# Attention tables on two engines, w loaded into its table, and SyncE waiting for the last scatters

## The reference

```python
for t in range(S):
    cur = np.einsum('bhd,bhe->bhde', u[None] * kt, vt)
    y[:, :, t] = np.einsum('bhd,bhde->bhe', rt, state + cur)
    state = w[None, :, :, None] * state + np.einsum('bhd,bhe->bhde', kt, vt)
...
skip_score = x @ w_skip; do_compute = skip_score > 0
e_idx = np.argmax(logits, axis=1); gate_w = probs[..., e_idx]
y = gate_w[:, None] * (np.maximum(x[rows of e] @ w1[e], 0) @ w2[e])
```

## Time and profile before

| | us |
|---|---|
| median of 3 runs | 607.92 |
| lowest and highest | 605.97, 608.97 |
| the profiled execution | 608.97 |
| its span, first to last instruction | 607.3 |
| TensorE busy | 559.0 (92%) |
| VectorE busy | 384.1 (63%) |
| GpSimd busy | 251.0 (41%) |
| ScalarE busy | 236.0 (39%) |
| mean granted clock of TensorE | 0.961 of full |

### The profile page before, as it was taken

The page is one execution under the profiler, slowest core; times in us unless marked ns, Lnnn a source line. Parts: engine busy times, 40 slices in busy tenths (PEclk is TensorE's granted clock), DMA queues, the critical chain, the costliest instruction groups (busy, mean ns, idle before and its releaser), DMA issues. The chain is left out here.

```text
span 607.3 us, 15679 instructions
## 1 busy us (share of the span) xinstructions
PE 559.0 (92%) x5618; PEld 532.4 (88%) x5619; DVE 384.1 (63%) x762; ACT 236.0 (39%) x567; POOL 251.0 (41%) x346
## 2 busy tenths in 40 slices
PE   3999999989799999999949779999999999999993
PEld 3899889968799999999938669999999999999992
DVE  5898888958777777777714745564647463737330
ACT  0233333324166565556605014362526351516220
POOL 5777778721443334443330033141524332324231
PEclk9899999987799999999979798999999999999997
DMA  9698899766377567666459111545264434111100
GB/s 141 105 188 159 160 167 166 144 248 209 123 248 229 164 219 242 216 190 189 123 147 361 35 50 47 200 137 192 71 223 159 149 138 148 48 40 44 39 15 25
DMA packets 114123, 89.54 MB, mean 147 GB/s; under 512 B 80672, under 2 KB 104931, under 8 KB 114080
## 3 DMA queue, kind: packets, MB, share of 16 engines
q1 hardware_dynamic: 106304, 74.16, 43.6%
q0 software_dynamic: 7776, 14.82, 8.8%
HBM read 80.44 MB, written 13.27 MB: 154 GB/s over the span
## 5 line engine op out<-in xcount | busy, mean ns | idle before, releaser
L814 DVE TENSOR_TENSOR w_lo<-w_raw,w_hi 128x384 fp32r<-128x384 f32 (+1 forms) x224 | 130.3, 608 | 6.2 <-ACT w_hi L809 2.4
L1079 PE MATMUL e_ps_h<-e_x_hi,w_hi 128*128 128x256 f32 (+2 forms) x384 | 122.3, 319 | 2.6 <-DVE e_x_lo L1179 2.6
L1080 PE MATMUL e_ps_h<-e_x_lo,w_hi 128*128 128x256 f32 (+2 forms) x384 | 122.0, 318 | 0.0
L1081 PE MATMUL e_ps_h<-e_x_hi,w_lo 128*128 128x256 f32 (+2 forms) x384 | 122.0, 318 | 0.0
L1079 PE MATMUL e_ps_y<-w_hi,e_h_hi 128*128 128x384 f32 (+1 forms) x344 | 119.5, 347 | 0.0
L809 ACT CAST w_hi<-w_raw 128x384 fp32r<-128x384 f32 (+1 forms) x224 | 118.1, 557 | 0.8 <-issue 0.5
L1155 ACT ACTIVATE e_h_hi<-e_ps_h 128x256 fp32r<-128x256 f32 (+1 forms) x128 | 59.5, 465 | 150.8 <-PE e_ps_h L1081 146.0
L1081 PE MATMUL e_ps_y<-w_hi,e_h_lo 128*128 128x384 f32 (+1 forms) x344 | 115.6, 336 | 0.0
L1080 PE MATMUL e_ps_y<-w_lo,e_h_hi 128*128 128x384 f32 (+1 forms) x344 | 115.2, 335 | 0.0
L1210 DVE SCALAR_TENSOR_TENSOR e_h_lo<-e_ps_h,e_h_hi 128x256 fp32r<-128x256 f32 (+1 forms) x128 | 66.9, 523 | 53.7 <-ACT e_h_hi L1155 51.9
L1079 PEld LDWEIGHTS e_ps_h<-e_x_hi,w_hi 128*128 128x128 f32 x384 | 74.0, 193 | 4.3 <-DVE e_x_lo L1179 3.1
(11 more groups left out here) (155 smaller groups left out, 829.4 us busy)
## 6 DMA issues: line engine op xcount, KB each, us to landing
w_raw<-in_moe_w_dram SPq DMA_DIRECT2D x32, 1536.0 KB, 6.6
r_in<-in_r_dram SPq DMA_DIRECT2D x24, 192.0 KB, 3.2
k_in<-in_k_dram SPq DMA_DIRECT2D x24, 192.0 KB, 3.9
v_in<-in_v_dram SPq DMA_DIRECT2D x24, 192.0 KB, 4.0
x_rows<-rows SPq DMA_DIRECT2D x24, 192.0 KB, 3.5
w_lo<-x_rows SPq DMA_DIRECT2D x6, 768.0 KB, 6.2
x_in<-x_rows,e_ent_in POOLq DMA_INDIRECT x33, 3.2
out_dram<-y_rows,e_ent_out POOLq DMA_INDIRECT x19
```

The source lines that it names most:

```text
L814: eng.tensor_tensor(self._of(self.lo1[par], self.lo2[par], n), self._of(self.raw1[par], self.raw2[par], n), self._of(self.hi1[par], self.h ...
L1079: pe.matmul(o, s_hi, m_hi, start=(k == 0), stop=False)
L1080: pe.matmul(o, s_hi, m_lo, start=False, stop=False)
L1081: return pe.matmul(o, s_lo, m_hi, start=False, stop=(k == last))
```

## The change

- **w and u.** ScalarE's queue loads both halves of w straight into `w_pow[:, 0, :]`, and u_row behind them; w has a semaphore of its own (`w_loaded`, 32) and so has u (`u_loaded`). The tile w_col and VectorE's copy are gone. SyncE's first loads are now r, k and v of step 0. VectorE's memsets clear w_pow's first column and w_g.
- **Clearing.** GpSimd clears only the 16 padding columns of each head in r_in and k_in.
- **shrink on GpSimd.** GpSimd builds the lower half of shrink by doubling, in six multiplications from the right end (1, 2, 4, 8, 16, 32 positions of four heads each), each waiting for the step before and for the power of w that it needs; a seventh multiplication makes the upper half, once VectorE has the reciprocal `grow[:, :, 0]`. It comes after the state memsets and ahead of ru. VectorE keeps the powers and grow (16 instructions that count, and not 20); its reciprocal and multiplication for shrink are gone, it waits for `shrunk` at 8 ahead of r_sc of step 0, and makes shrink_up behind k_sc of step 0.
- **TensorE** turns shrink_up behind the scores of step 0 instead of ahead of the turning of step 1.
- **Semaphores of the loads.** `loaded` becomes `rk_loaded` and `v_loaded`; TensorE's turning and GpSimd's ru wait for r and k alone, TensorE's state update and GpSimd's bonus_v for v.
- **Gate weights.** SyncE's wait for VectorE's memset of w_g stands just ahead of the loads of w_g.
- **Routing.** e_iota is made first and has its own semaphore, which the candidates wait for; the wait for the other constants stands ahead of the limits.
- **Last scatters.** In both mixtures SyncE loads the number of tiles and waits for the scatters; in the second it then counts up a semaphore that nobody reads. GpSimd's load of that number and its wait are gone; its wait for the gathers stays.

The names of the semaphores and the counts that follow from them are left out of the diff below.

```diff
@@ -37,7 +37,10 @@
     HD = H * D
-    TABLE_STEPS = 20
+    HALF = P // 2
+    POWERS = [1, 1, 2, 3, 4, 5]
+    LOW = 8
+    TABLE_STEPS = 16
@@ -53,7 +56,6 @@
-        w_col = sb("w_col", [P, NP])
@@ -113,11 +115,6 @@
-            sp.wait_ge(dve_zeroed, 2)
-            for j in range(2):
-                sp.dma_start(w_col[PAD * j:PAD * j + D, :], w.rearrange("(n j) d -> j d n", j=2)[j], allow_slow_non_contiguous=True).then_inc(small, 16)
-            sp.dma_start(u_row[:], u.rearrange("h d -> (h d)").partition_broadcast(P)).then_inc(small, 16)
@@ -135,12 +132,13 @@
                 for dst, src in ((r_in, r), (k_in, k)):
-                    sp.dma_start(dst[b][:, :, 0:D], src[b, :, bass.ds(t0, P), :].rearrange("h t d -> t h d")).then_inc(loaded[b], 16)
-                sp.dma_start(v_in[b][:], v[b, :, bass.ds(t0, P), :].rearrange("h t d -> t h d")).then_inc(loaded[b], 16)
+                    sp.dma_start(dst[b][:, :, 0:D], src[b, :, bass.ds(t0, P), :].rearrange("h t d -> t h d")).then_inc(rk_loaded[b], 16)
+                sp.dma_start(v_in[b][:], v[b, :, bass.ds(t0, P), :].rearrange("h t d -> t h d")).then_inc(v_loaded[b], 16)
...
                 step(0, sub)
+            sp.wait_ge(dve_zeroed, 2)
@@ -157,8 +155,8 @@
             for n in range(B):
-                pool.memset(r_in[n][:], 0.0).then_inc(zeroed, 1)
-                pool.memset(k_in[n][:], 0.0).then_inc(zeroed, 1)
+                pool.memset(r_in[n][:, :, D:PAD], 0.0).then_inc(zeroed, 1)
+                pool.memset(k_in[n][:, :, D:PAD], 0.0).then_inc(zeroed, 1)
@@ -168,13 +166,23 @@
+            pool.memset(shrink[:, :, HALF - 1:HALF], 1.0).then_inc(shrunk, 1)
+            for n in range(6):
+                m = 2 ** n
+                pool.wait_ge(shrunk, n + 1)
+                pool.wait_ge(tables, POWERS[n])
+                pool.tensor_tensor(shrink[:, :, HALF - 2 * m:HALF - m], shrink[:, :, HALF - m:HALF], w_pow[:, n, :].unsqueeze(2).to_broadcast([P, NP, m]), ALU.mult).then_inc(shrunk, 1)
+            pool.wait_ge(shrunk, 7)
+            pool.wait_ge(tables, LOW)
+            pool.tensor_tensor(shrink[:, :, HALF:P], shrink[:, :, 0:HALF], grow[:, :, 0:1].to_broadcast([P, NP, HALF]), ALU.mult).then_inc(shrunk, 1)
             pool.wait_ge(consts, 2 + B)
-            pool.wait_ge(small, 48)
+            pool.wait_ge(u_loaded, 16)
...
-                pool.wait_ge(loaded[b], 48 * (c + sub // 4 + 1))
+                pool.wait_ge(rk_loaded[b], 32 * (c + sub // 4 + 1))
@@ -196,11 +205,15 @@
+            act.wait_ge(dve_zeroed, 1)
+            for j in range(2):
+                act.dma_start(w_pow[PAD * j:PAD * j + D, 0, :], w.rearrange("(n j) d -> j d n", j=2)[j], allow_slow_non_contiguous=True).then_inc(w_loaded, 16)
+            act.dma_start(u_row[:], u.rearrange("h d -> (h d)").partition_broadcast(P)).then_inc(u_loaded, 16)
...
             act.wait_ge(consts, 2 + B)
-            act.wait_ge(tables, 8)
+            act.wait_ge(tables, 7)
@@ -250,10 +263,9 @@
                 dve.wait_ge(tables, done[0])
-            dve.memset(w_col[:], 1.0).then_inc(dve_zeroed, 1)
+            dve.memset(w_pow[:, 0, :], 1.0).then_inc(dve_zeroed, 1)
             dve.memset(w_g[:], 0.0).then_inc(dve_zeroed, 1)
-            dve.wait_ge(small, 48)
-            link(dve.tensor_copy(w_pow[:, 0, :], w_col[:]))
+            dve.wait_ge(w_loaded, 32)
@@ -263,10 +275,6 @@
-            link(dve.reciprocal(shrink[:, :, 0:P // 2], grow[:, :, 1:P // 2 + 1]))
-            link(dve.tensor_tensor(shrink[:, :, P // 2:P], shrink[:, :, 0:P // 2], grow[:, :, 0:1].to_broadcast([P, NP, P // 2]), ALU.mult))
-            link(dve.tensor_tensor(shrink_up[:], shrink[:], w_pow[:, 7, :].unsqueeze(2).to_broadcast([P, NP, P]), ALU.mult))
@@ -292,7 +300,9 @@
+            dve.wait_ge(shrunk, 8)
             rk(0, 0)
+            dve.tensor_tensor(shrink_up[:], shrink[:], w_pow[:, 7, :].unsqueeze(2).to_broadcast([P, NP, P]), ALU.mult).then_inc(tables, 1)
@@ -372,16 +382,12 @@
-            pe.wait_ge(tables, TABLE_STEPS)
-            for p in range(NP):
-                ins = pe.transpose(ps_x[:, P * p:P * p + P], shrink_up[:, p, :], ident[:])
-            ins.then_inc(tab_ps, 1)
...
+                c0, sub0 = c, sub
@@ -395,6 +401,11 @@
                 ins.then_inc(scored, 1)
+                if isinstance(i, int) and i == 0:
+                    pe.wait_ge(tables, TABLE_STEPS + 1)
+                    for p in range(NP):
+                        ins = pe.transpose(ps_x[:, P * p:P * p + P], shrink_up[:, p, :], ident[:])
+                    ins.then_inc(tab_ps, 1)
@@ -559,15 +571,15 @@
         def _(pool):
+            pool.iota(e_iota[:], [[1, E]], base=0, channel_multiplier=0, allow_small_or_imprecise_dtypes=True).then_inc(e_made, 1)
...
             pool.memset(keep[:], 1.0).then_inc(made, 1)
-            pool.iota(e_iota[:], [[1, E]], base=0, channel_multiplier=0, allow_small_or_imprecise_dtypes=True).then_inc(made, 1)
...
-            pool.wait_ge(made, 5)
+            pool.wait_ge(made, 4)
@@ -698,7 +710,7 @@
             link(dve.tensor_tensor(eq[:], logits, top_all, ALU.is_equal))
-            dve.wait_ge(made, 7)
+            dve.wait_ge(e_made, 1)
@@ -714,6 +726,7 @@
             count = seen[:, :, TILES - 1:TILES].to_broadcast([P, E, LIMITS])
+            dve.wait_ge(made, 6)
@@ -861,7 +874,7 @@
         h_ready = sem("h_ready"); h_hi_done = sem("h_hi_done"); h_lo_done = sem("h_lo_done")
-        y_ready = sem("y_ready"); y_done = sem("y_done")
+        y_ready = sem("y_ready"); y_done = sem("y_done"); all_stored = sem("all_stored")
@@ -963,10 +976,14 @@
                     follow(pairs - 1, par, 1, par)
-                end = sp.value_load(starts[0:1, E:E + 1], min_val=1, max_val=top)
-                sp.wait_ge(scattered, 16 * (end + 1))
+            end = sp.value_load(starts[0:1, E:E + 1], min_val=1, max_val=top)
+            sp.wait_ge(scattered, 16 * (end + 1))
+            if m == 0:
                 load_next(sp)
+            else:
+                sp.sem_inc(all_stored, 1)
@@ -1042,11 +1059,8 @@
             run_experts(pool, expert)
-            end = pool.value_load(starts[0:1, E:E + 1], min_val=1, max_val=top)
...
-            if m == 1:
-                pool.wait_ge(scattered, 16 * (end + 1))
```

14 lines of the change are left out of this document (8 added, 6 removed).

## The result

| | before | after |
|---|---|---|
| median of 12 runs each, us | 606.47 | 601.43 |
| lowest and highest | 604.09, 609.27 | 598.41, 603.80 |
| ratio, 95% interval | | 0.9914 (0.9891 to 0.9938) |
| the profiled execution, its span | 608.97, 607.3 | 600.54, 598.8 |
| mean granted clock | 0.961 | 0.976 |

The change takes 5.2 us off (3.8 to 6.6). The forecast was 601.6, a gain of 6.3. That the time fits to 0.2 us is in part luck, because two errors cancel: the gain was about 1 us smaller, and the median that it was taken from, 607.92 of three runs, was about 1.4 above that of twelve. Three prices of the sum have to be judged apart: 3.2 at the start, 0.3 in routing, 2.8 at the end.

The account below looks back on a forecast made before the run. TensorE was taken as busiest, its work in the two mixtures left alone. Gains of 3.2 (start), 0.3 (routing) and 2.8 (end) sum to 6.3 us, from 607.92 to 601.6; range 599.5 to 605.0.

Parts of the forecast that it names:

- w and k_in: First loads: w lands at 3.9 us (bounds 3.4 and 5.2), k_in of step 0 near 6.5 instead of 7.9.
- VectorE's chain: Tables on VectorE: 3.7 us from w to the end of grow instead of 5.0, so grow is complete at 7.6.
- GpSimd's chain: State memsets end near 4.7 us; seven shrink steps take 2.9, so shrink is there at 7.7 (bounds 1.3 and 7.6).
- The chains meet: VectorE and GpSimd holding each other up adds 1.0 us; r_sc of step 0 starts near 8.7 instead of 15.21.
- TensorE to k_end: Turning, warm-ups, scores, table: k_end of step 0 at 14.5 us, not 16.59; masks of step 1 at 21.5; gain 3.2.
- Routing: First routing: VectorE's 0.32 us idle ahead of its candidates goes; gain 0.3, nothing in the second routing.
- The last scatters: Kernel end: GpSimd's DRAIN starts behind the last scatter's issue, near 599.2 us; gain 2.4 to 3.3, taken as 2.8.
- The clock at step 1: Rival: TensorE's idle gap comes before step 1's turning; start gains 1.0, total 4.1, time 603.8 us; chance 0.12.
- The DRAIN that does not move: Rival at the end: DRAIN's length follows the scatter's landing; total gain 3.5, time 604.4 us; chance 0.07.
- the one that ends with the scatter: Rival at the end: SyncE's 601.0 decides; with the start at its best, 599.5 us; chance 0.04.
- The first-use cost: Rival: GpSimd's first tensor_tensor stands before it works; if r_sc starts at 13.7, total gain nothing, 607.8 us; chance 0.04.
- The slower case: Rival: VectorE and GpSimd lock each other step by step, shrink at 17.8 us; 3.7 slower, 611.6; chance 0.03.

Follow-up runs that it names:

- after_again: The changed kernel once more, unaltered, for a second profile of its start; one profile, 600.99 us.
- shrink_on_vector: The changed kernel, but VectorE makes shrink as before and GpSimd's seven steps are gone; 604.14 us, 0.9957 of the kernel before.
- one_warmup: The changed kernel with 8 TensorE warm-up transposes in place of 16; 602.47 us, 0.9913 of the kernel before.
- u_late: The changed kernel with u_row loaded by SyncE behind r, k and v of step 0; 600.07 us, 0.9887 of the kernel before.
- turn_table_first: The changed kernel with shrink_up turned right behind the warm-ups, ahead of step 1's turning; 599.36 us, 0.9882 of the kernel before.
- tail_undone: The changed kernel with GpSimd again waiting for the last scatters in the second mixture; 601.81 us, 0.9942 of the kernel before.
- ru_behind_grow: The changed kernel with GpSimd's ru and ruk of step 0 waiting for all of VectorE's grow; 601.91 us, 0.9915 of the kernel before.
- no_scatter: The changed kernel without the second mixture's scatters, except the first into the spare row; one profile, 597.88 us.
- tail_alone: The kernel before with only the wait for the last scatters moved from GpSimd to SyncE; 604.72 us, 0.9978 of the kernel before.

## Why the prediction was right or wrong, point by point

What ties these runs together is k_end(0) and masks(1), in the profiles that keep GpSimd's order of steps:

| kernel | k_end(0) | masks(1) | apart |
|---|---|---|---|
| after | 16.44 | 23.18 | 6.74 |
| after_again | 15.35 | 22.09 | 6.74 |
| shrink_on_vector | 16.48 | 23.23 | 6.75 |
| one_warmup | 15.56 | 22.29 | 6.73 |
| u_late | 14.86 | 21.61 | 6.75 |
| turn_table_first | 13.61 | 20.36 | 6.75 |

Tail_undone, ru_behind_grow and no_scatter give 6.74 as well. Whatever moved k_end(0), by up to 2.9 us, the masks of step 1 followed to 0.02. In the kernel before they lay 8.17 behind it (tail_alone: 8.08), with TensorE at the low clock. So the start's gain has two parts: 1.4 from this shorter distance, which goes with the clock that TensorE kept, and only 0.15 and 1.24 in the two profiles of after from an earlier k_end(0). That the order of TensorE's work is not what shortened the distance is seen in turn_table_first, which turns the table first again and has 6.75.

1. *w and k_in.* w at 3.9: the powers began at 4.33 to 4.55 over the profiles, within the bounds (3.4 to 5.2), late by half a microsecond. **k_in near 6.5 was wrong**: TensorE began at 7.47 and 7.63. I priced two queues sharing the transfers at 0.5 for w, and at nothing for k. u_late shows the missing term: u_row, sent ahead, costs k 1.5 us.
2. *VectorE's chain.* Grow alone from w: predicted 3.7; from 4.55 to 8.67 in ru_behind_grow, 4.1. Near; 0.3 of the rest is the step of 64 elements.
3. *GpSimd's chain.* 2.9 predicted, 2.7 measured (4.78 to 7.50), shrink at 7.50 against 7.7. The price of 0.18 + 0.0021 n was good: 0.20 for 4 elements, 0.41 for 128, 0.66 for 256.
4. *The chains meet.* 1.0 predicted; 1.5 came from ru and ruk, which I had down as the cause of the long steps before but not in this sum, and some 0.3 from the shrink steps. r_sc was at 10.09 and 9.89, past the 9.8 that I gave as its latest; it cost nothing, because the warm-ups lasted to 12.8. The Trainium skill (SBUF — State Buffer, Who interferes with whom) states that a VectorE instruction with two SBUF inputs contends with a GpSimd instruction that reads SBUF, and not with one that only writes it. The traces agree at two places: beside GpSimd's state memsets, which only write, the first power was not held, and ru and ruk, which read, held the long grow steps. In the second profile of after, VectorE and then GpSimd:

```profile
4.38 1.14 DVE L270 TENSOR_TENSOR w_pow<-w_pow 128x4 f32<-128x4 f32 x6 [3.23 <-DMA w_pow<-in_w_dram]
...
3.11 1.49 POOL L167 MEMSET state<- 128x384 f32 x4
```

   The powers start at 4.38, while the last memset runs until 4.6, and the six take 1.14, what they took behind the memsets in the kernel before. Ru and ruk held the two grow steps of 128 and 256 elements by 0.7 each. At a third place the rule does not show: GpSimd's first shrink steps, which read SBUF too, run beside the later powers from 4.73 on (4.78 in the first profile), and the six still take 1.14.
5. ***TensorE to k_end* is the step that failed.** 14.5 predicted, 16.44 and 15.35 measured. Of the 1.9 in the first profile, 1.0 is k's landing (7.47 and not 6.5) and 0.9 the spacing of the transposes: the warm-ups 3.62 and not 3.03, and the first four of step 1 still at the slow pace. In the second profile k's landing alone costs 1.1, more than the whole miss of 0.85, and the warm-ups were shorter than forecast. So the term that failed in both is the load of k, where u_row's transfer was priced at nothing. What stands behind k_end was right: 3.82 to ruk(1)'s end against 3.8, and 2.9 from the sum to the masks against 3.1. I had allowed for a fall of the clock in TensorE's gap; it did not come. So the start gave 1.6 and 2.7 in the two profiles, and not 3.2; with tail_undone (22.80) and no_scatter (22.26), which have the same start, the mean of four is 2.2. The recorded bound of 3.7 ("w at 3.4, nothing held") does not follow from its own part 4, by which r_sc may be as late as 9.8 before anything moves: an earlier w gains nothing there.
6. *Semaphores.* Nothing seen apart from point 5.
7. *Routing.* No idle ahead of the candidates. From the routing's first instruction on GpSimd to the table it took 17.54 and 17.57 in the two kernels with the old code, 17.23 and 17.37 in two profiles of after: 0.2 to 0.3. Right.
8. *The last scatters.* The DRAIN began 0.9 behind the issue, as predicted, and ran beside the scatter. It took 5.42 or 5.43 in all kernels that have the scatters and this order: the lower end of my 2.4 to 3.3, not the middle. The 4.48 that I averaged in belongs to the first mixture, whose DRAIN took 4.45 to 5.28 over the profiles. Mis-sized by 0.4.

Sum by the traces: 2.2 (the mean of four) + 0.25 + 2.4 = 4.9, inside the measured 3.8 to 6.6; what the first mixture and the second routing may add is not in it. The range held, but its ends do not follow from the recorded terms: with the DRAIN ended by 601.0 (6.0 in place of 2.8), a start of 3.7 and 0.3 the best case is 597.9 and not 599.5, and with a start of 1.0, 0.3 and 2.4 the poor one is 604.2 and not 605.0.

*The rivals.* The clock at step 1 did not fall by its record, but a relative of that rival came: the faster pace set in late, which cost the same stage 0.9 in the first profile of after and nothing against the forecast in the second. The DRAIN that does not move, and the one that ends with the scatter, both fell. The first-use cost did not show: GpSimd's first multiplication ran at once behind its memset, at 4.78, in 0.20. The Trainium skill (GPSIMD Engine Reference, Instruction dispatch) states about 6 us for the first call of a freshly loaded kernel; no profile here shows any of it, nor whether a kernel was freshly loaded. The slower case fell with the same row.

## What to carry to other kernels

When work leaves an engine's chain, follow the first consumer on the longest line, here GpSimd's k_end behind TensorE's table, and ask what now stands ahead of it. An order that was good when the tables were late can be wrong when they are early: moving four transposes gave 2.0 to 2.5 us at the masks of step 1, as much as the whole start of the change (2.2). A large load that nobody waits for soon should not be issued ahead of the one that everything waits for. And a wait can be taken off an engine whose end-of-block DRAIN is long, if another engine with a short one can hold it.
